# A fused attention and two-MLP kernel: how its first two head pairs are loaded, rotated and fed to TensorE

## What is computed

```python
x1, x2 = x[..., :half], x[..., half:]               # rotary step on q and k, [4, 8, 576, 64]
rot = concatenate([x1 * cos - x2 * sin, x1 * sin + x2 * cos], -1)
scores = matmul(q_rot, k_rot.T) / 8                  # per head, 576 x 576
attn = exp(scores - max(scores)); attn = attn / (sum(attn) + 1e-09)
a = matmul(attn, v)                                  # -> [4, 576, 512]
x = a + relu(layernorm(a) @ w_ch1) @ w_ch2           # hidden size 2048
u, v = split(gelu(x @ w_in)); v = w_sg @ layernorm(v) + b_sg
out = x + (u * v) @ w_out
```

## Time and profile before

| | us |
|---|---|
| median of 3 executions | 928.74 (928.68 to 928.8) |
| the profiled execution | 927.43 |
| its span in the profile | 925.6 |
| TensorE busy | 903.8 (98%) |
| VectorE, ScalarE, GpSimd busy | 703.3, 543.5, 558.7 |

### The profile page before, as it was taken

The page is one execution under the profiler, slowest core; times in us unless marked ns, Lnnn a source line. Parts: engine busy times, 40 slices in busy tenths (PEclk is TensorE's granted clock), DMA queues, the critical chain, the costliest instruction groups (busy, mean ns, idle before and its releaser), DMA issues.

```text
span 925.6 us, 18234 instructions
## 1 busy us (share of the span) xinstructions
PE 903.8 (98%) x6153; PEld 838.6 (91%) x6153; DVE 703.3 (76%) x1149; ACT 543.5 (59%) x1184; POOL 558.7 (60%) x552
## 2 busy tenths in 40 slices
PE   4999999999999999999999999999999999999998
PEld 3899999999999889999899889899988989989897
DVE  4899899999999899933767788789998572664623
ACT  3899999999998666633655555465565222202110
POOL 4989898998977567575666668758976210010100
PEclk9999999999999999999999999999999999999999
DMA  6243334334323233000000000001300001010011
GB/s 182 69 101 94 82 93 97 82 93 98 85 66 91 85 111 104 23 1 1 1 1 1 1 1 1 1 17 54 109 9 1 1 1 46 1 55 4 1 47 57
DMA packets 49737, 45.51 MB, mean 49 GB/s; under 512 B 18880, under 2 KB 39616, under 8 KB 49536
## 3 DMA queue, kind: packets, MB, share of 16 engines
q1 hardware_dynamic: 49232, 44.26, 17.5%
q10 hardware_dynamic: 432, 0.30, 0.1%
HBM read 28.81 MB, written 4.72 MB: 36 GB/s over the span
## 4 chain that ended last, share of the span: by engine, by line
PE 87%; DVE 7%; ACT 2%; DMA 1%; issue 1%; SPq 1%; ACTq 0%; DVEq 0%
PE fc_ps L2158 16%; PE seven_ps L2188 14%; PE ring_ps L2054 8%; PE scores_ps L1990 6%; PE wide_ps L2357 6%; PE bank_ps L2313 6%; PE wide_ps L2336 6%; PE bank_ps L2371 5%; PE ring_ps L2001 5%; PE seven_ps L2238 2%; DVE lefts L1664 2%; PE seven_ps L2158 2%; PE scores_ps L1983 2%; DVE hid_sums L1652 2%; PE ring_ps L1936 2%
## 5 line engine op out<-in xcount | busy, mean ns | idle before, releaser
L2158 PE MATMUL fc_ps<-xT,W1s 128*128 128x512 f32 (+1 forms) x828 | 191.0, 379 | 0.4 <-ACT hid L1171 0.3
L2188 PE MATMUL seven_ps<-rights,lefts 128*128 128x256 f32 x1344 | 173.6, 284 | 0.0
L2188 PEld LDWEIGHTS seven_ps<-rights,lefts 128*128 128x128 f32 x1344 | 169.5, 191 | 4.4
L2158 PEld LDWEIGHTS fc_ps<-xT,W1s 128*128 128x128 f32 x828 | 146.2, 189 | 27.7 <-ACT hid L1171 1.3
L1477 DVE TENSOR_REDUCE nmax<-scores_ps 128x1 f32<-128x576 f32 x144 | 106.4, 749 | 15.9 <-PE scores_ps L1990 10.6
L970 POOL TENSOR_TENSOR rights<-w_rest,rights 128x256 fp32r<-128x256 f32 x84 | 80.9, 963 | 54.6 <-ACT rights L1214 54.6
L1077 ACT ACTIVATE E<-scores_ps,nmax 128x576 f32<-128x576 f32 x128 | 95.6, 748 | 10.2 <-DVE nmax L1477 9.5
L1032 POOL TENSOR_TENSOR rstd<-ve,power 128x1 f32<-128x1 f32 x18 | 14.5, 807 | 138.7 <-DVE ve L1846 138.7
L1486 DVE TENSOR_TENSOR prob_lo<-ring_ps,prob_hi 128x512 fp32r<-128x512 f32 x144 | 95.3, 681 | 2.2 <-ACT prob_hi L1091 1.7
L1990 PE MATMUL scores_ps<-stack 128*128 128x288 f32 x384 | 89.4, 319 | 1.4 <-DMA swapped_k<-stack 1.0
L1091 ACT ACTIVATE prob_hi<-ring_ps 128x512 fp32r<-128x512 f32 x144 | 85.4, 612 | 4.1 <-PE ring_ps L2001 3.3
(11 more groups left out here) (187 smaller groups left out, 2070.4 us busy)
## 6 DMA issues: line engine op xcount, KB each, us to landing
swapped_k<-stack SPq DMA_DIRECT2D x32, 144.0 KB, 2.4
stack<-stack SPq DMA_DIRECT2D x32, 144.0 KB, 2.4
w_raw<-in_w SPq DMA_DIRECT2D x18, 256.0 KB, 2.9
qk_raw<-in_k SPq DMA_DIRECT2D x16, 256.0 KB, 2.7
v_raw<-in_v SPq DMA_DIRECT2D x16, 256.0 KB, 2.8
qk_raw<-in_q SPq DMA_DIRECT2D x15, 256.0 KB, 2.8
w_rest<-in_w SPq DMA_DIRECT2D x7, 512.0 KB, 4.1
out<-out_sb SPq DMA_DIRECT2D x14, 256.0 KB, 2.3
```

What stands on the lines that cost most here:

```text
L2158: mm = nc.tensor.matmul(fc1_bank(n, f)[:, 0:cols], W1s[:, slot1(f), w, c, :], xT[:, x, c, 0:cols], start=first, stop=(c == DC - 1 and x == 1))
L2188: mm = nc.tensor.matmul(seven_ps[k][:, 2 * P * a:2 * P * (a + 1)], lefts[:, k, x, P * a:P * (a + 1)], rights[:, k, w, :], start=(g == 0 an ...
```

## The change

It has seven parts.

1. First transfers: the small table of pair 0 moves from SyncE's queue to the head of ScalarE's. SyncE starts with pair 0's k, then the unit matrix, and then waits for that k to land before it starts any transfer of pair 1; pair 1's k and its table now come before q and its table.
2. The two tail transfers of a `load` of q or k become one, for all pairs.
3. `first_rope` uses buffers of its own, cut out of `E`. GpSimd's work for pair 1 now waits for `first_lo[0][0]` (low part of q, head 0) and no longer for head 1's.
4. Pair 1's high parts are made by ScalarE (`second_high`, from the sum in `rot`), so GpSimd's order for that pair is scale, crosses, both adds, then both lows.
5. K1 is made before Q1 in every round, K1 before score tile 0, Q1 behind it.
6. The tails of head 1's swapped keys get a semaphore of their own, for which only the second half of score tile 4 waits.
7. TensorE multiplies zeros (128x512, `idle`) at its start and in rounds -1 and 0.

```diff
@@ buffers
+        first_turned = E[:, 0, :].rearrange("p (w t d) -> p w t d", w=2, d=D)
+        first_crossed = E[:, 1, :].rearrange("p (w t d) -> p w t d", w=2, d=D)
+        zeros = stack[:, 1, QMAIN[0]:QMAIN[0] + MAIN]
@@ load
-            for h in range(2):
-                eng.dma_start(dst[TAIL * h:TAIL * (h + 1), NT, :],
-                              src[bass.ds(p.i * 2 + h, 1), NT * P:S, :].rearrange("h p d -> p (h d)")).then_inc(done, 16)
+            eng.dma_start(dst[:, NT, :], src[bass.ds(p.i * 2, 2), NT * P:S, :]).then_inc(done, 16)
@@ block.sync
-            sp.dma_start(first_rotary, first_dram).then_inc(first_table_in, 16)
             load(sp, pair(0), 1)
             sp.dma_start(ident[:, :], eye_dram).then_inc(ident_in, 16)
-            for which in range(2):
+            sp.wait_ge(qk_in[0][1], 32)
+            for which in (1, 0):
                 sp.dma_start(rotary[:, which].rearrange("p a t d -> p (a t d)"), table_dram[:, which]).then_inc(table_in[which], 16)
                 load(sp, pair(1), which)
@@ block.gpsimd: scale, crosses
-                    pool.wait_ge(first_lo[1][which], 1)
+                    pool.wait_ge(first_lo[0][0], 1)
@@ qk_high
-                if not live(p) or is_round(p, 0):
+                if not live(p) or is_round(p, 0) or is_round(p, 1):
                     return
@@ add
+                if is_round(p, 1):
+                    pool.wait_ge(rope_step, last_of(rope_order, p, [(step, which) for step in ("scale", "cross0", "cross1")], 1))
+                else:
+                    pool.wait_ge(split_hi[which], p.i)
@@ qk_low
+                if is_round(p, 1):
+                    pool.wait_ge(split_hi[which], 1)
@@ block.scalar
+            def second_high(r, which):
+
+                if not is_round(r, 0):
+                    return
+                act.wait_ge(rope_step, count(rope_order, r + 1, ("add", which), 1))
+                wait_filled(act, r, ("QK"[which], 0), ("QK"[which], 1), ("TL", 0))
+                nc.scalar.activation(qk_split[:, which, :, 0:D], rot[:, which], ACT.Copy).then_inc(split_hi[which], 1)
+
+            act.dma_start(first_rotary, first_dram).then_inc(first_table_in, 16)
             load(act, pair(0), 0)
...
                 exp(r, 2)
+                second_high(r, 1)
...
                 exp(r, 3)
+                second_high(r, 0)
                 v_high(r)
@@ block.vector
+            nc.vector.memset(zeros.bitcast(f32), 0.0).then_inc(zeroed_stack, 1)
@@ block.tensor: score, s == NT
                     for half in range(2):
+                        if half == 1:
+                            pe.wait_ge(tails_swapped[p.odd], p.i * 24 + (48 - 24 * p.odd))
@@
+            def idle(count):
+
+                for _ in range(count):
+                    nc.tensor.matmul(ring_ps[0][:, :], zeros[:, 0:P], zeros, start=True, stop=True)
+
+            pe.wait_ge(zeroed_stack, 1)
+            idle(16)
             pe.wait_ge(ident_ready, 1)
```

More of the change, by code:

```diff
@@ L286, in attention_and_mlps @@
         keys_swapped = [[sem(f"keys_swapped{h}{odd}") for odd in range(2)] for h in range(2)]
+        tails_swapped = [sem(f"tails_swapped{odd}") for odd in range(2)]
         scores = sem("scores")
@@ L1418, in first_scale @@
                 n = tiles.stop - tiles.start
-                nc.vector.scalar_tensor_tensor(out=rot[:, which, tiles, :], in0=raw_tiles(pair(0), which)[:, tiles, :], scalar=factor,
+                nc.vector.scalar_tensor_tensor(out=first_turned[:, which, tiles, :], in0=raw_tiles(pair(0), which)[:, tiles, :], scalar=factor,
                                                in1=first_cos[:, 0:n], op0=ALU.mult, op1=ALU.mult).then_inc(first_rot, 1)
@@ L1959, in wait_stacks @@
                 for h in heads:
-                    count = 16 if h == 0 else 40
-                    pe.wait_ge(keys_swapped[h][p.odd], p.i * count + (2 * count - count * p.odd))
+                    pe.wait_ge(keys_swapped[h][p.odd], p.i * 16 + (32 - 16 * p.odd))
             def score(p, s):
@@ L2093, in body @@
                 make_stack_tails(r)
+                if is_round(r, 0):
+                    idle(3)
                 score(r - 1, 7)
@@ L2100, in body @@
                 make_stack(r, 0, 0)
+                if is_round(r, 0):
+                    idle(3)
                 score(r - 1, 8)
-                make_stack(r, 1, 0)
+                make_stack(r, 1, 1)
+                if is_round(r, 0):
+                    idle(3)
                 transpose_group(r - 1, 1, 0)
@@ L2113, in body @@
                 score(r, 1)
+                if is_round(r, 0):
+                    idle(2)
                 transpose_tails_of_both(r - 1)
@@ L2124, in body @@
                 transpose_group(r, 0, 2)
+                if is_round(r, 0):
+                    idle(1)
                 times_v(r - 1, 0, 0, range(2, NTT))
@@ L2132, in body @@
                 make_stack(r + 1, 0, 1)
+                if is_round(r, -1):
+                    idle(2)
             def hidden(n, f):
```

36 lines of the change are left out of this document (18 added, 18 removed), and 6 rows, old and new, of tables (RING_JOBS, filled_order).

## The result

| | before | changed |
|---|---|---|
| median of 20 runs each, us | 928.36 | 926.39 |
| ratio to before, 95% interval | | 0.9979 (0.9973 to 0.9985) |
| profiled execution / its span, us | 927.43 / 925.6 | 925.61 / 923.8 |

What follows compares the result with a forecast made beforehand. TensorE, busy 98% of the span, was taken as the bound, with early gains judged by ScalarE's first high part of probabilities. Buffers +1.25, zero products +0.15 and K1/tails -1.2 gave +0.2: 928.9 us, range 924.5 to 930.9.

Steps and rivals of the forecast that it cites:

- The reference point: ScalarE's first high part of probabilities (G2), at 24.68 us; its shift was taken as the shift of the kernel's end.
- is close behind ScalarE: Rest of round 1, after TensorE goes on at 26.0: claimed to follow ScalarE closely; no size given.
- Own buffers, +1.25: Start: GpSimd beside VectorE holds first_rope until 19.0, not 11.9, putting ScalarE's first high part 1.25 us later.
- They go one for one: During first_rope: VectorE and GpSimd instructions alternate, seven VectorE instructions being held, 9.2 us in all.
- First transfers, -1.1 and -0.5: Start: pair 0's k lands 1.1 us sooner; first swap can start at 10.95 against 11.42, score tile 0 at 14.3.
- The 6.2 us that I laid behind the wait: SyncE's queue after pair 0's k lands: 11 transfer starts, 6.2 us, before the first swap can start.
- High parts on ScalarE: Round 0: pair 1's high parts put 1.4 us on the path; GpSimd's side costed at nothing, 0.5 if cover fails.
- Zero products, +0.15: Early TensorE: worth 0.5 us on tiles 0 and 2, but possible slow clock after a pause adds 0.15.
- My doubt of the clock: TensorE idle from 11 to 16.3 before tile 0: doubted that the clock stays up; half of 0.4 us charged.
- K1 first, tails apart, -1.2: Rounds 1, 4 and 5: TensorE's waits before score tile 4 vanish, gaining 1.2 us; bounds 0 and -1.5.
- GpSimd is hardly in the way: Faster rival at first_rope: VectorE nearly through or not held, -2.6 at the start, 924.9 in all; chance 0.38.
- A cast is passed over: Slower rival at first_rope: GpSimd's next instruction precedes a waiting VectorE cast, costing 1.4; 930.3 to 931.7; chance 0.15.

Runs made afterwards that it cites:

- e14: Changed kernel with GpSimd waiting again for the whole of first_rope (second head's low part) before pair 1's work; 926.63 us.
- e8: Changed kernel plus three extra GpSimd sums of zeros run beside VectorE's first_rope; 925.2 us in one run.
- e1: Changed kernel with two 16 KB tail transfers per load of q and k again, in place of the merged one; 924.5 us.
- e13: Changed kernel with the earlier kernel's first transfers: table first on SyncE, two tail transfers per load, no SyncE wait, old pair 1 order; 923.2 us.
- e7: Changed kernel with pair 1's high parts made by GpSimd again instead of ScalarE; 925.99 us.
- e10: Changed kernel with two tail transfers per load again and pair 1's high parts on GpSimd again; 925.66 us.
- e4: Changed kernel without any zero products on TensorE; 928.0 us.
- e6: Kernel before the change plus only TensorE's zero products and the memset they read; 927.8 us.
- e5: Kernel before the change plus only K1 ahead of Q1 and the tails' own semaphore; 926.19 us.
- e2: Changed kernel without SyncE's wait for pair 0's k; 926.16 us.
- e11: Changed kernel with two tail transfers per load again and each of ScalarE's high parts one exponential earlier; 924.26 us.

## Why the prediction was wrong

*The reference point.* "Whatever moves that instruction moves the end, as long as nothing else is later." Something was later. By G2 and T0 the changed kernel is 0.51 us worse, and my sum followed only that way. I had the earlier trace rows in hand, cited them for a rival, and did not ask who waited behind that VectorE instruction: TensorE did, and GpSimd's pause-free stream was a second way, to 42.87 us, that ended last in round 1. The chain that ended last even passed through that instruction (41.20, 1.71 us); of this stretch my text says only that round 1 "is close behind ScalarE". This is the step that turned the sign. With two high parts taken out of that stream GpSimd ended 0.88 sooner and T1 moved by -0.44, in spite of the worse start; the slack of TensorE's way (44.27 against 43.54) swallowed the start's loss. That GpSimd also started 1.9 us sooner did not count: what it gained went into the wait of 2.61 us for ScalarE, and in e14, without the earlier start, GpSimd's low parts are done at 41.12, sooner than the changed kernel's 41.99.

*Own buffers, +1.25.* Wrong in size and in its mechanism. "They go one for one" holds once GpSimd is in (e8: 1.21 to 1.39), but a stream that is already running keeps the newcomer out until its first gap. GpSimd came at 11.39, not at 9.8, and entered at about 12.22 (an estimate: its end less 1.40), when six of the seven instructions that I had it hold had begun. In e1 it came at 10.68 and entered at 12.13 all the same. The Trainium skill, SBUF — State Buffer, "Who interferes with whom", has "Whoever issues first gets the shared pair for the whole instruction"; it says so of VectorE's two-port modes, and of VectorE instructions with two SBUF inputs that they contend with GpSimd ones that read SBUF. The trace agrees for a single instruction of the second kind (the held one took 1.53 us, its like at 11.72 took 0.42). What the rule doesn't say, and these runs show, is that the next instruction of the first engine also goes ahead of the waiting one. The shared buffers had not been the bound before either: GpSimd's first product for k waited in the code only for the low part of k for head 1, done at 12.30, and began at 13.25 when k had landed.

*First transfers, -1.1 and -0.5.* The mechanism was wrong. k landed 0.17 sooner; tile 0 started 2.2 later. The 6.2 us that I laid behind the wait were 7.5 (5.68 to 13.21), 1.4 of it v's start at 1.98, and the swap's flight grew from 2.74 to 3.14. I had costed the merged transfer as one start saved. e1 puts its true price at 1 to 2 us, e13 that of both transfer parts together at some 3 in the medians, a part of which is the clock.

*High parts on ScalarE.* I laid 1.4 us on the path; e7 shows 0.31 in T0, or 0.73 from the start of tile 0 on (e10 against e1: 0.47 and 0.63). The rest lies in waits for a maximum. What they take off GpSimd I costed at nothing; e10 against e1 shows 0.64 in T1.

*Zero products, +0.15.* My doubt of the clock was right for the profiled execution (0.57 after the pause) and not for e14's (1.00), and the pause was not the reason I took it for: in e13 the clock fell without it. Their worth in T0 is 0.96 here (e4) and 1.44 on the kernel before (e6), where it reaches the end for hardly anything.

*K1 first, tails apart, -1.2.* This held: 1.29 between T1 and the far point, 1.25 in e5. The number is partly luck, since 0.3 of my 1.2 belonged to round 1, ahead of T1; the two later waits, which I had at 0.96 with their pipeline, were worth 1.19. In the medians the part is worth 2.0 alone; 0.38 of that, in the profiles, is a T1 that moved with pair 1's k (GpSimd started at 12.76 there, 13.25 before), which nothing in the part explains, and the rest is open. A mean of several profiles would be needed to share it out.

*The rivals.* "GpSimd is hardly in the way" was what happened on VectorE, but its -2.6 at the start did not follow, since the transfers lost it. "A cast is passed over" was nearly the true finding about rinv, read as an accident: it is no matter of chance, since VectorE's TENSOR_SCALAR ended 0.03 to 0.04 after GpSimd's stream in twelve kernels (before, the changed kernel, e1, e2, e5 to e10, e13 and e14), and took 0.15 us in e11, where that stream had already ended.

## What to carry to other kernels

Before following one chain, look for an engine that works through the same stretch without any pause, and for the short instruction of another engine that ends exactly when it does; the path can be there although no row names that engine as what was waited for. Price every part against both ways: here a part worth 1.44 us at one point was worth next to nothing at the end, until another part had moved the other way. And run the parts singly: the best kernel is the change without its first two parts, which concern the transfers. Before two single executions are compared, look where each had its low granted clock.

## What was not expected of the hardware

- A GpSimd instruction that reads SBUF, issued beside a VectorE stream of two-input instructions without gaps, took 2.23 to 3.27 us instead of 1.40, and got in (by its end less 1.40) 0.15 to 0.19 us after the start of the cast that precedes VectorE's wait for its own result, in all ten kernels in which it came before that cast. A nine-column TENSOR_SCALAR of VectorE took 0.15 us alone and up to 2.88 us beside GpSimd's gapless stream.
- One start of a transfer on SyncE's queue took 1.98 us instead of 0.59 where one 32 KB transfer of tails stood in place of two of 16 KB. All seven kernels with merged tails show it, with 1.63 to 3.30 us, and none of the ten with two tails does. The runs don't show why.
- After a pause of over 3 us in front of tile 0, TensorE's granted clock read 0.57 in one execution and 1.00 in another with the same start of tile 0; in e13 it read 0.50 ahead of tile 0 without such a pause, TensorE having been busy since 9.59.
